# Two units' attention outputs issued between the broadcasts of the third, with wider dummy matmuls and pairs of PSUM banks as one operand

## The reference

```python
def _attn_ref(q, k, v, i_gate, f_gate, o_gate):
    ...
    for t in range(S):
        m_new = np.maximum(f_gate[:, :, t] + m, i_gate[:, :, t])
        f_stab = np.exp(f_gate[:, :, t] + m - m_new)
        i_stab = np.exp(i_gate[:, :, t] - m_new)
        m = m_new
        C = f_stab * C + i_stab * np.einsum('bhd,bhe->bhde', vt, kt)
        n = f_stab * n + i_stab * kt
        h_tilde = np.einsum('bhde,bhe->bhd', C, qt)
        denom = np.maximum(np.abs(n . qt), 1.0)
        y[:, :, t] = sigmoid(o_gate[:, :, t]) * h_tilde / denom

h = x @ w_in;  x = np.maximum(0.01 * h, h) @ w_out
h = x @ w2_in; out = (h * np.cos(h)) @ w2_out
```

## Time and profile before

| | us |
|---|---|
| median of 3 runs | 813.08 (812.62 to 813.42) |
| the profiled execution | 816.6 |
| its span, first to last instruction | 814.6 |
| TensorE busy | 801.0 |
| VectorE busy | 620.7 |
| ScalarE busy | 465.9 |
| GpSimd busy | 302.2 |
| mean granted clock of TensorE | 0.993 |

### The profile page before, as it was taken

How to read it: one execution, slowest core, us unless ns; L and a number is a source line. 1 busy time by engine, 2 the same in 40 slices (tenths; PEclk the granted TensorE clock), 3 DMA queues, 4 the chain that set the end, 5 groups by cost and what they waited for, 6 DMA issues and landing times.

```text
span 814.6 us, 19415 instructions
## 1 busy us (share of the span) xinstructions
PE 801.0 (98%) x7657; PEld 781.0 (96%) x7657; DVE 620.7 (76%) x1371; ACT 465.9 (57%) x1036; POOL 302.2 (37%) x304
## 2 busy tenths in 40 slices
PE   8899999999999999999999999999999999999998
PEld 6889999999999999999999999999999999999998
DVE  8578877776776777777644688888888888888896
ACT  5354434433434444434356777767676777777776
POOL 4666434222222432222026643333333333434343
PEclk9899999999999999999999999999999999999999
DMA  9586323433223344240034401110010202020000
GB/s 325 190 248 211 124 100 119 165 135 141 96 94 144 124 157 144 95 158 31 2 117 126 165 2 50 72 50 25 20 54 1 74 1 73 1 73 1 3 23 25
DMA packets 34329, 76.63 MB, mean 94 GB/s; under 512 B 3776, under 2 KB 17600, under 8 KB 34240
## 3 DMA queue, kind: packets, MB, share of 16 engines
q1 hardware_dynamic: 34192, 75.35, 27.2%
q10 hardware_dynamic: 48, 0.05, 0.0%
HBM read 63.39 MB, written 11.99 MB: 93 GB/s over the span
## 4 chain that ended last, share of the span: by engine, by line
PE 91%; DVE 5%; ACT 2%; issue 1%; DMA 1%; POOL 0%; DVEq 0%; ACTq 0%
PE h L704 33%; PE acc L717 13%; PE acc L719 13%; PE acc L718 12%; PE s L704 10%; PE x L680 2%; PE s L644 2%; DVE r_f L1305 2%; PE s L621 2%; PE s L658 1%; PE s L673 1%; DVE r_f L1303 1%; DMA raw_in<-w1i 1%; PE acc L803 1%; DVE g_f L1313 0%
## 5 line engine op out<-in xcount | busy, mean ns | idle before, releaser
L704 PE MATMUL h<-xT,w_in 128*128 128x384 f32 x1536 | 307.0, 342 | 1.7 <-DVE w_in L1369 1.2
L704 PEld LDWEIGHTS h<-xT,w_in 128*128 128x128 f32 x1536 | 267.2, 188 | 4.1 <-DVE w_in L1369 1.4
L880 ACT ACTIVATE t_f<-h 128x384 f32<-128x384 f32 x192 | 94.1, 490 | 275.1 <-PE h L704 275.0
L717 PE MATMUL acc<-w_out,g_hi 128*128 128x320 f32 x756 | 237.2, 314 | 0.7 <-POOL g_lo L1578 0.3
L719 PE MATMUL acc<-w_out,g_lo 128*128 128x320 f32 x756 | 233.6, 309 | 0.0
L718 PE MATMUL acc<-w_out,g_hi 128*128 128x320 f32 x756 | 232.3, 307 | 0.0
L1578 POOL TENSOR_TENSOR g_lo<-g_f,g_hi 128x384 fp32r<-128x384 f32 x123 | 125.9, 1024 | 203.9 <-ACT g_hi L880 203.9
L1293 DVE TENSOR_TENSOR g_f<-h,t_f 128x384 f32<-128x384 f32 x128 | 71.2, 556 | 115.4 <-ACT t_f L880 115.4
L717 PEld LDWEIGHTS acc<-w_out,g_hi 128*128 128x128 f32 x756 | 142.0, 188 | 2.0 <-issue 1.1
L718 PEld LDWEIGHTS acc<-w_out,g_hi 128*128 128x128 f32 x756 | 142.1, 188 | 0.0
L719 PEld LDWEIGHTS acc<-w_out,g_lo 128*128 128x128 f32 x756 | 141.8, 188 | 0.0
(11 more groups left out here) (157 smaller groups left out, 789.4 us busy)
## 6 DMA issues: line engine op xcount, KB each, us to landing
kvo_s<-kvo SPq DMA_DIRECT2D x24, 566.0 KB, 6.3
qk_s<-qk SPq DMA_DIRECT2D x24, 512.0 KB, 5.1
x_dram<-stage SPq DMA_DIRECT2D x8, 960.0 KB, 4.5
xT<-x_dram SPq DMA_DIRECT2D x8, 960.0 KB, 4.9
qe<-q SPq DMA_DIRECT2D x24, 256.0 KB, 4.0
D<-g_dram SPq DMA_DIRECT2D x42, 128.0 KB, 2.9
eG_b<-e_dram SPq DMA_DIRECT2D x42, 128.0 KB, 3.1
out<-x SPq DMA_DIRECT2D x24, 160.0 KB, 1.8
```

The lines of the kernel that those rows point to most:

```text
L704: last = nc.tensor.matmul(bank[:, 0:BLOCK], w(a), x[:, k, :], start=(n == 0), stop=(n == 7))
L717: nc.tensor.matmul(acc[t][:, 0:DM], hi[:, r], w_out[:, 0, j, :], start=(j == 0), stop=False)
L880: copy = lambda o, i, **k: nc.scalar.activation(o, i, ACT.Copy, **k)
```

## The change

TensorE's list: within and carried of unit 0 move up behind the state products of unit 1, ahead of the spreads of unit 2; within and carried of unit 1 move ahead of the state products of unit 2. The dummies at the second place go, and the counts at three others change. Up to four dummies are issued as one matmul of up to 512 columns against the same weights. VectorE's list: normaliser(0,0) and normaliser(0,1) come before state(0,2), and outputs(0,0) before sigmoid(0,2,1). GpSimd's list: gated(0,0) comes before first_scaled(2). The banks of acc, h and s are declared as tensors of several banks each, in the same places, and probs, first_probs, normaliser, normalised and outputs work on both banks of a unit in one instruction; this holds for all 24 units.

```diff
-WARM = (5, 2, 3, 1, 8, 4)
+WARM = (5, 0, 4, 1, 6, 4)
...
-        def bank(name):
-            return ctx.enter_context(nc.psum_tensor(name, [P, 512], F32))
+        def banks(name, n):
+            return ctx.enter_context(nc.psum_tensor(name, [P, n, 512], F32))
...
+        acc_banks, h_banks, s_banks, x_banks = banks("acc", TILES), banks("h", 2), banks("s", 2), banks("x", 1)
...
+        def unit_pair(b, c):
+            return (s_banks, h_banks, acc_banks[:, 0:2, :])[c] if first(b, c) else s_banks
...
             def warm_up(n, bank):
 
-                for _ in range(n):
-                    nc.tensor.matmul(bank[:, 0:P], ident[:, :], ident[:, :], start=True, stop=True)
+                while n > 0:
+                    k = min(n, 4)
+                    nc.tensor.matmul(bank[:, 0:k * P], ident[:, :], ident[:, :].unsqueeze(1).to_broadcast([P, k, P]), start=True, stop=True)
+                    n -= k
...
             unit_state(0, 1)
+            unit_within(0, 0)
+            unit_carried(0, 0)
             spread_decays(2)
             spread_keys(2)
             unit_scores(0, 2)
             pe.wait_ge(cols_done, 1)
             spread_scales(2)
-            unit_state(0, 2)
-            unit_within(0, 0)
-            unit_carried(0, 0)
             unit_within(0, 1)
             unit_carried(0, 1)
-            warm_up(WARM[1], acc[2])
+            unit_state(0, 2)
             unit_within(0, 2)
             unit_carried(0, 2)
             warm_up(WARM[2], acc[2])
...
-                for e in range(2):
-                    d = D[:, c % BUFS, 2 * e:2 * e + 2, :]
-                    last = tt(d, unit_banks(b, c)[e][:, 0:2 * CHUNK].rearrange("p (h t) -> p h t", h=2), d, ALU.mult)
-                last.then_inc(P_done, 1)
+                d = D[:, c % BUFS, :, :].rearrange("p (e h) t -> p e (h t)", e=2)
+                tt(d, unit_pair(b, c)[:, :, 0:2 * CHUNK], d, ALU.mult).then_inc(P_done, 1)
...
-                for o, x in zip(sums, parts):
-                    last = ts(x, o, -1.0, 1.0, ALU.mult, ALU.max)
-                last.then_inc(nrm_step, 1)
+                sums, parts = output_heads(b, c)[:, :, :, HD], nrm[:, p, :].rearrange("p (e h) -> p e h", e=2)
+                ts(parts, sums, -1.0, 1.0, ALU.mult, ALU.max).then_inc(nrm_step, 1)
                 dve.wait_ge(nrm_step, n * 2 + 1)
-                for o, x in zip(sums, parts):
-                    last = tt(x, o, x, ALU.max)
-                last.then_inc(nrm_step, 1)
+                tt(parts, sums, parts, ALU.max).then_inc(nrm_step, 1)
...
             state(0, 1)
+            normaliser(0, 0)
             sigmoid(0, 1, 1)
             first_probs(2)
+            normaliser(0, 1)
             sigmoid(0, 2, 0)
             state(0, 2)
-            normaliser(0, 0)
-            normaliser(0, 1)
+            outputs(0, 0)
             sigmoid(0, 2, 1)
-            outputs(0, 0)
             outputs(0, 1)
...
             second_rates()
+            gated(0, 0)
             first_scaled(2)
-            gated(0, 0)
             gated(0, 1)
```

More of the change, by code:

```diff
@@ L148, in build @@
         G_s = [t_f[0:GH, 0, :], t_f[0:GH, 1, :]]
[L150 to L153, removed]
+        acc_banks, h_banks, s_banks, x_banks = banks("acc", TILES), banks("h", 2), banks("s", 2), banks("x", 1)
+        acc = [acc_banks[:, t, :] for t in range(TILES)]
+        h_bank = [h_banks[:, k, :] for k in range(2)]
+        s_bank = [s_banks[:, k, :] for k in range(2)]
+        x_bank = x_banks[:, 0, :]
         ring_bank = h_bank + s_bank
@@ L1172, in first_probs @@
                 dve.wait_ge(dx_done, c + 1)
[L1173 to L1176, removed]
+                d = D[:, c, :, :].rearrange("p (e h) t -> p e (h t)", e=2)
+                tt(d, unit_pair(0, c)[:, :, 0:2 * CHUNK], d, ALU.mult).then_inc(ph_done, 1)
             def first_keys():
@@ L1185, in first_keys, with output_heads @@
                    ALU.mult).then_inc(kw0_done, 1)
-            def output_heads(b, c, e):
-                return unit_banks(b, c)[e][:, OUT:OUT + SIDE * VD].rearrange("p (h d) -> p h d", h=SIDE)
+            def output_heads(b, c):
+                return unit_pair(b, c)[:, :, OUT:OUT + SIDE * VD].rearrange("p e (h d) -> p e h d", h=SIDE)
             def normaliser(b, c):
@@ L1193, in normaliser @@
                 dve.wait_ge(O_done, n + 1)
-                sums = [output_heads(b, c, e)[:, :, HD] for e in range(2)]
-                parts = [nrm[:, p, SIDE * e:SIDE * (e + 1)] for e in range(2)]
-                for o, x in zip(sums, parts):
-                    last = ts(x, o, -1.0, 1.0, ALU.mult, ALU.max)
-                last.then_inc(nrm_step, 1)
+                sums, parts = output_heads(b, c)[:, :, :, HD], nrm[:, p, :].rearrange("p (e h) -> p e h", e=2)
+                ts(parts, sums, -1.0, 1.0, ALU.mult, ALU.max).then_inc(nrm_step, 1)
                 dve.wait_ge(nrm_step, n * 2 + 1)
-                for o, x in zip(sums, parts):
-                    last = tt(x, o, x, ALU.max)
-                last.then_inc(nrm_step, 1)
+                tt(parts, sums, parts, ALU.max).then_inc(nrm_step, 1)
                 dve.wait_ge(nrm_step, n * 2 + 2)
@@ L1208, in normalised @@
                 dve.wait_ge(nrm_done, unit(b, c) + 1)
[L1209 to L1212, removed]
+                o, x = output_heads(b, c)[:, :, :, 0:HD], nrm[:, c % 2, :].rearrange("p (e h) -> p e h", e=2)
+                tt(o, o, x.unsqueeze(3).to_broadcast([P, 2, SIDE, HD]), ALU.mult).then_inc(normed_done, 1)
             def by_gate(b, c):
@@ L1232, in outputs @@
                     n = HD - d
-                    o = output_heads(b, c, 1)
+                    o = output_heads(b, c)[:, 1]
                     tt(x1[:, p, DM:DM + n], o[:, h - SIDE, d:HD], gate[:, h, d:HD], ALU.mult)
                     tt(x1[:, p, DM + n:DM + REM], o[:, h + 1 - SIDE, 0:HD], gate[:, h + 1, :], ALU.mult)
[L1236 to L1240, removed]
+                tt(x1[:, p, 0:DM].rearrange("p (e h d) -> p e h d", e=2, h=SIDE), output_heads(b, c)[:, :, :, 0:HD],
+                   gate.rearrange("p (e h) d -> p e h d", e=2), ALU.mult).then_inc(x1_done, 1)
             def state(b, c):
```

## The result

The changed kernel takes 816.45 us (median of 7 executions, 814.87 to 817.21) against 813.08 of before (7 executions, 812.28 to 813.90): ratio 1.0033, 95% interval 1.0019 to 1.0047. The forecast was 811.8, so the sign was wrong, and the time lies above the range; it moved by more than the 3 us from which on the prediction calls itself wrong altogether. The profiled executions alone mislead: the profiled execution of the changed kernel took 815.64 us with a span of 813.6, less than the 814.6 of the one profiled execution of before. That one had been slow for its kernel, 3.5 us over the median. Of 121 executions of before that ran beside the experiments (one more, disturbed, took 862.25 us at a mean clock of 0.85 and is left out), 61 had a mean granted clock of 0.999 or more and 21 one of 0.996 or less; only three had 0.993, as the profiled one did.

A forecast was written before the change was run, and what follows sets the result against it. TensorE, busy 801.0 of 814.6 us, was taken as the bound. A first product 1.05 us sooner plus 0.25 at 77 us made 1.3: 816.6 to 815.3, less 3.5 to the median, 811.8 us; range 809.3 to 814.3.

The forecast's parts named there:

- I subtract the same: 811.8: Last step: profiled execution 816.6 us would become 815.3; the median lay 3.5 us lower, so the same was subtracted.
- my 34.45: End of the head: forecast start of the first product on TensorE, 1.05 us sooner than the profiled 35.50.
- The wait that the change adds: Head, unit 2: state(0,2) ends at 26.7, TensorE idle from 24.1, within(0,2) at 26.7 instead of 25.75; costs 1.0 us.
- Four in one instruction ... 1.07 us: Head dummies at low clock: four in one instruction load weights once per pass, 1.07 us against 1.7 one by one.
- rival D: Wider dummies and merged operands fail to save: 0.9 + 0.3 of 1.3 us come back, 813.0; 0.18 together with B.
- The end of the block falls ... in carried(0,1): TensorE's code block ends after carried(0,1)'s first few matmuls, at 21.8; halt there until a restart at 23.0.
- my 16.7: Time at which TensorE begins the code block before the expected halt in the new order, instead of 17.5.
- The clock of the first 7 us: Start of the head: first dummies, 0.6 us shorter in all, push towards slower ahead of an idle 1.4 us.
- rival C: Slower: moved loads delay the code block to 25.8, state(0,2) behind unit 1's outputs; 813.4 or 815.1 us; chance 0.14.
- Pairs of banks: VectorE's two-bank operands save 0.3 us per unit; TensorE gains 0.25 us at the 77 us wait.
- B: Gain swallowed at 50.6 us, where TensorE waits for the same load; 0.3 stays, 812.8 us; 0.18 together with rival D.

The follow-up runs named there:

- a_fill: Changed kernel with six dummies added before the first spreads, where TensorE is idle: 815.01 us, ratio 1.0013.
- a_keep: Changed kernel with ten dummies added in TensorE's wait for unit 2's state, ahead of within(0,2): 815.31 us, ratio 1.0019.
- b_order: Kernel before with only the new order of TensorE, VectorE and GpSimd, without the second place's dummies: 815.76 us, ratio 1.0023.
- before_again: Kernel before once more, unchanged in what it does, for a second trace: 813.90 us, ratio 0.9995.
- a_state_back: Changed kernel with unit 2's state products and VectorE's state(0,2) put back ahead of unit 1's outputs and normaliser(0,1): 813.44 us, ratio 0.9997.
- b_wide: Kernel before with only the dummies issued up to four at a time, counts as before: 813.99 us, ratio 0.9992.
- b_dense: Kernel before with 24 small matmuls where the change puts unit 0's outputs, nothing moved: 821.01 us, ratio 1.0083.
- b_fill: Kernel before with six more dummies between hide_later and the first spreads: 812.42 us, ratio 0.9986.
- b_pairs: Kernel before with only the pairs of banks as one VectorE operand: 813.86 us, ratio 1.0003.
- c_best: Kernel before, old order, with pairs of banks, wide dummies in new counts and six dummies before the first spreads: 813.26 us, ratio 0.9989.

## Why the prediction was wrong

**"I subtract the same: 811.8"** is the first step that failed. It carried a difference from one execution of before to the median. The profiled one had a halt of 1.78 us, two stretches at half clock and its first product at 35.50; the six traces of the old order have it between 32.14 and 35.50, so my 34.45 was no gain over them. The 3.5 us between the profiled time and the median were in front of me; I explained them by nothing. That I had 815.3 us for the profiled execution and it took 815.64 is luck: its first product came 2.6 us later than I said, and what made up for it is the low stretch at 52.7 that this trace did not have. The changed kernel's profiled execution lay 0.8 us under its median, not 3.5 over it.

**"The wait that the change adds"** was right in kind and size: TensorE idle for 2.6 us expected, 2.74 measured, in both traces. But I priced it at 1.0 us: within(0,2) at 26.7 against 25.75. The 26.7 was right where the first spreads ran at full clock, as in the trace that I forecast from: 26.76 in a_fill, 26.71 in a_keep. The 25.75 was not a fair other side. In the five traces of the old order with such first spreads within(0,2) starts without a wait at 24.48 and 24.49, where the halt in unit 0's carried took 0.8 and 0.7 us, and at 25.49 to 25.75, where the halt ahead of it took 1.6 to 1.8. So the price lay between 1.0 and 2.3 us, and I took the lowest. With the first spreads at half clock within(0,2) started at 28.11, 28.72 and 29.16 (b_order) against 26.08 (before_again), 2.0 to 3.1 us later. With the wait comes a lower clock: none of 19 executions of the changed kernel had a mean clock of 0.999 or more, half of before's had. Whether it falls right behind the wait differs (27.4 in one trace, 40.9 in the other). a_state_back shortens this wait to 0.9 us, and the loss is gone.

Where the first product's 2.6 us beyond the forecast come from, in the first trace: 1.4 lie ahead of within(0,2), mostly the first spreads at half clock (unit 1's spreads at 13.70, not 12.05), the halt of 0.60 that I did not have, and 1.2 back for the halt in carried(0,1) that I had and that did not come. The other 1.15 lie behind it (8.90 us to the first product, forecast 7.75), of which 0.8 are the price of the wide dummies. (ScalarE's three steps behind unit 1's transposes add up to 32.8, not 32.7; that moves the sum by 0.1 at the most.)

**"Four in one instruction ... 1.07 us"** was wrong. The changed kernel's instruction with four dummies (two records, at low clock) started at 29.98 and the transposes behind it at 31.85: 1.87 us where I had 1.07; the price of four narrow ones, 1.7, would have been nearer. The 0.107 us of "weight load" in a narrow dummy is none: a record of 128 columns starts 0.213 us after the one before, a record of 512 columns 0.85, four times as long, so nothing is left for a load that is paid once per record. b_wide: no difference. This is the first half of rival D, which had too small a chance; its second half, that the merged operands do not do what they should, did not hold.

**"The end of the block falls ... in carried(0,1)"** missed a halt and had one that did not come. The block before it ends at TensorE's record 449 (matmuls, weight loads and waits counted in their order), which the new order reaches inside within(0,0). In all 16 traces TensorE went on from record 449 5.8 to 7.1 us after it had gone on from record 193; my 16.7 was only 5.3 after 11.45. The trace of before shows the stretch from 11.45 to 17.49, where 128 matmuls and 128 weight loads took 6.0 us of unbroken work. Unit 0's outputs have 96 instructions in 0.8 us, and TensorE is through the block early and stands, while the DMA engines are full:

```profile
11.53:18.61 7.08, 5.23 (x133) 4.23 (x133) 5.86 (x16) 4.53 (x10) 4.63 (x6) 1.00 1.05 381
```

(a_state_back: 7.08 us, of which TensorE was busy 5.23.) In that kernel the halt cost nothing in the median, so it is not the loss. At record 705, in carried(0,1), where I had a halt of 1.2 us, neither trace of the changed kernel has one. That these halts come behind every 256th record held in every trace (449, 705, 961), and that they are waits for code can now be said with more than their place: in all 23 of them a packet of 16,384 bytes of the instruction queue landed 1.2 to 1.7 us before TensorE went on. The rule of the Trainium skill (Runtime: NRT & Kernel Launch, Instruction fetch mechanics) that crossing a block is mostly hidden did not hold in this head: every trace has at least one such halt of 0.5 us or more.

**The clock of the first 7 us.** I named the first dummies under rival C as a push towards slower. Where the clock rises differs from one execution to the next, for the old width as for the new: first spreads at low clock in before_again, b_order and b_dense too. What more dummies there do is shown by b_fill.

**Pairs of banks.** The wait at 77 us went from 0.81 to 0.53, as forecast. In the median 0.3 us cannot be told (b_pairs 1.0003).

**The rivals.** C had the place right (state(0,2) behind unit 1's outputs) and the sign, at 0.14. Its trigger was wrong: it made the moved loads responsible, and set the turning point at a restart of 25.3, where the wait needs no late block at all. B, a gain swallowed at 50.6, is answered by the traces: from the first product to TensorE's restart near 85 us it is 48.7 to 49.1 us where the product comes after 35.3 and 49.4 to 49.8 where it comes sooner (without the three traces that have more, 51.0, 51.3 and 53.4, all with a low stretch in between). b_fill's product was 3.2 us sooner than c_best's (32.14 and 35.34), its restart 2.6 us sooner (81.61 and 84.23). So well under 1 us of a sooner head is lost there, and the rest comes through.

## What to carry to other kernels

Before a sum is made against a trace, hold its time against the median of the runs: where it stands apart, each halt and each low stretch in it needs a reason to be there in most executions, or a second trace. An order in which TensorE must wait for a chain on another engine at a fixed place can be worse than one with slack there, even if the idle times of one profile look alike: here the wait came in every trace of the order, while the halts that the old order had in its place were long in some and short in others. Issue the work that feeds the longest chain (here the state products of unit 2 and VectorE's state) first, and what only fills (normaliser, reciprocal) behind.

## What the runs showed of the hardware

- A float32 matmul on the full array against 128 columns of weights shows as two records, at low clock 0.213 us each for 128 columns and 0.85 for 512 (first dummies of before and of the changed kernel). Packing dummies into one instruction saved instructions and no time (b_wide 0.9992).
- With the DMA engines at 1.04 to 1.07, no trace passed the 256 TensorE records from 193 to 449 in under 5.8 us (5.8 to 7.1 in 16 traces). Dense short instructions halted at their end, by 0.6 to 1.9 us, and TensorE went on 1.2 to 1.7 us after a packet of 16,384 bytes of the instruction queue had landed (23 halts).
- Executions of before with a mean clock of 1.000 took 812.8 us in the median (47 of 121), those with 0.993 took 817.6 (three). With dummies in the idle 1.1 to 1.4 us before the first spreads, these ran at full clock in five of five traces; without, in five of eleven.
